# A first MLP layer by Strassen's seven products on three 768-token tiles, with its weights streamed through HBM

## The chip, the cores and the metric

One core of one Trainium2 chip. The metric is the device time of one execution, in microseconds (us). A kernel's time is the median of its runs; one more execution is taken with the hardware profiler.

## The reference

A windowed attention (4 batches, 8 heads of 64, 768 positions, chunks of 32 queries against 8 memory and 56 context keys) gives x of 3072 tokens by 512. Two MLPs follow:

```python
h = np.maximum(np.maximum(x @ w1, x @ w2), x @ w3)     # 512 -> 768
y = h @ w_out                                          # 768 -> 512
h = y @ w_in                                           # 512 -> 2048
g = np.where(h >= 1, h, np.where(h <= -1, 0.0, (h + 1) ** 2 / 4))
out = g @ w_out2                                       # 2048 -> 512
```

All is float32. The kernel splits each operand into a high part of type fp32r and a low part (value minus high part) and takes three matmuls for each product: high-high, low-high, high-low.

## The kernel before

The five engines run their own instruction lists, written out by hand, in order, and meet only in semaphores; nothing is scheduled by a planner.

**Tiles and first MLP.** TT = 384 tokens are a tile, TILES = 8. `tile_a` (TensorE's L541, VectorE's L896, ScalarE's L715) does one tile: for each of six blocks f of 128 hidden columns, three products (w1, w2, w3) of 4 x 3 matmuls each, `layer1` (L495), into the three PSUM banks `mlp[0..2]`. ScalarE copies the first (`h_first`, L699), VectorE takes the maximum with the second and third (L880, L886), ScalarE makes h's high part and VectorE its low part (L892). Then `layer2` (L524): four outputs of 6 x 3 matmuls, copied by ScalarE (`y_out`, L708) and stored to `y_scratch` by SP. All weights of this MLP stay in SBUF. A tile is 216 + 72 matmuls of 384 columns.

**Attention.** 24 groups of 128 tokens. Three are done ahead; each tile of the first seven carries the three groups of the next between its products: `scores` (L449), softmax on VectorE and ScalarE (L839, L858, L674), `transposes` (L460), `weighted_v` (L476), and x's high and low parts straight out of PSUM (L695, L871). q, k and v come in by SP, three groups deep.

**Second MLP.** Tiles of TU = 768 tokens, four of them (u), each with PAIRS = 8 periods: 32 periods g. A period takes one pair of hidden blocks by Strassen: seven products of 2 x 3 matmuls on sums of weight blocks and of y blocks (`product`, L596), alternating between two banks, with the six down-projection outputs of earlier periods between them (`down`, L626: 6 matmuls of 512 columns each). VectorE combines the products (L982 to L1006), ScalarE and VectorE apply the activation and split g (L782, L794, L1008, L1014). y's sums and parts for the next u are made in periods 2 to 6 (L751, L934, L951).

**Weights of the second MLP.** POOL (`split_w_in` L365, `split_w_out` L398) makes the sums and the high and low parts, one item after another through one staging area, while the first MLP runs; SP brings the raw item and stores the result (L271, L278). In the second MLP POOL issues the load of each period's set: `wi` (L416, 1792 KB, two buffers) when the period two before has ended, `wo` (L419, 1024 KB) when its down products have. The loop is L430 to L438.

## Time and profile before

| what | value |
|---|---|
| median of 3 runs | 984.15 us (984.12 to 984.52) |
| profiled execution | 983.69 us |
| its span, first to last instruction | 981.6 us |
| TensorE busy | 968.8 us, 99% |
| VectorE, ScalarE, POOL busy | 48%, 36%, 15% |
| DMA moved | 181.52 MB, 185 GB/s over the span |

The profile books each matmul from its start to a modelled end, and those overlap, so the pace is read from starts. PEld is TensorE's weight load, DVE VectorE, ACT ScalarE, SPq and POOLq the engines as issuers of DMAs. The time outside the span, here 2.1 us, is start and end of the execution.

### The profile page before, as it was taken

What the parts mean: (1) busy time and instruction counts of PE and PEld (TensorE: products, weight loads), DVE (VectorE), ACT (ScalarE), POOL (GpSimd) and SP (SyncE); (2) the same over time, 40 slices, a digit from 0 to 9 for tenths busy, and PEclk for the clock granted to TensorE, in tenths of its full rate; (3) what the DMA queues carried; (4) which work ended last, traced back from release to release, by engine and by line L of the source; (5) the groups of instructions that cost most, each with busy time, mean ns of one, the idle gap of its engine ahead of it and who ended that gap; (6) DMA issues with size and microseconds to landing.
All of it is one profiled execution on the core that took longest, in us unless ns stands there. A gap on an engine that the chain in (4) does not pass through costs nothing.

```text
span 981.6 us, 18566 instructions
## 1 busy us (share of the span) xinstructions
PE 968.8 (99%) x7968; PEld 905.1 (92%) x7968; DVE 469.6 (48%) x713; ACT 354.5 (36%) x553; POOL 150.0 (15%) x176
## 2 busy tenths in 40 slices
PE   6999999999999999999999999999999999999998
PEld 5999999999999999999998888988888888888887
DVE  4662524244252434425456655566545666454452
ACT  3342212222222222222353625545354544444253
POOL 2022442405235230000000000000000000000000
PEclk9999999999999999999999999999999999999999
DMA  9462753645465361042735566655756545575532
GB/s 363 186 234 70 267 183 128 252 144 188 162 236 183 153 231 61 1 172 65 269 131 217 203 220 215 204 196 200 249 191 236 192 161 196 187 258 170 198 118 108
DMA packets 32206, 181.52 MB, mean 185 GB/s; under 512 B 3456, under 2 KB 7552, under 8 KB 21888
## 3 DMA queue, kind: packets, MB, share of 16 engines
q0 software_dynamic: 9216, 92.28, 27.0%
q1 hardware_dynamic: 22912, 88.09, 24.4%
q8 instruction: 63, 1.03, 0.4%
q14 instruction: 15, 0.12, 0.0%
HBM read 144.70 MB, written 35.65 MB: 184 GB/s over the span
## 4 chain that ended last, share of the span: by engine, by line
PE 98%; DMA 1%; DVE 0%; ACT 0%; issue 0%; SPq 0%
PE mlp_ps L491 23%; PE mlp_ps L492 23%; PE mlp_ps L493 23%; PE attn_ps L493 3%; PE scores_ps L493 3%; PE attn_ps L492 3%; PE scores_ps L492 3%; PE attn_ps L491 3%; PE scores_ps L491 3%; PE attn_ps L484 3%; PE scores_ps L457 2%; PE trans_ps L493 2%; PE trans_ps L492 2%; PE trans_ps L491 1%; PE trans_ps L466 1%; DMA qk_raw<-qk_l 1%
## 5 line engine op out<-in xcount | busy, mean ns | idle before, releaser
L491 PE MATMUL mlp_ps<-x_hi,w_hi 128*128 128x384 f32 x572 | 195.1, 341 | 0.0
L493 PE MATMUL mlp_ps<-x_lo,w_hi 128*128 128x384 f32 x572 | 191.5, 335 | 0.0
L492 PE MATMUL mlp_ps<-x_hi,w_lo 128*128 128x384 f32 x572 | 191.2, 334 | 0.0
L492 PE MATMUL mlp_ps<-yc,wi 128*128 128x384 f32 x448 | 150.7, 336 | 0.0
L493 PE MATMUL mlp_ps<-yc,wi 128*128 128x384 f32 x448 | 149.6, 334 | 0.0
L491 PE MATMUL mlp_ps<-yc,wi 128*128 128x384 f32 x448 | 149.6, 334 | 0.0
L787 ACT ACTIVATE ramp<-up,half_col 128x768 f32<-128x768 f32 x64 | 60.1, 939 | 197.4 <-DVE up L1004 178.2
L491 PEld LDWEIGHTS mlp_ps<-x_hi,w_hi 128*128 128x128 f32 x572 | 107.4, 188 | 1.9
L492 PEld LDWEIGHTS mlp_ps<-x_hi,w_lo 128*128 128x128 f32 x572 | 107.5, 188 | 0.0
L493 PEld LDWEIGHTS mlp_ps<-x_lo,w_hi 128*128 128x128 f32 x572 | 107.4, 188 | 0.0
L492 PEld LDWEIGHTS mlp_ps<-yc,wi 128*128 128x128 f32 x448 | 84.1, 188 | 8.8
L491 PEld LDWEIGHTS mlp_ps<-yc,wi 128*128 128x128 f32 x448 | 84.1, 188 | 8.1 <-DVE up L1002 0.3
L672 ACT ACTIVATE h_hi<-h_max 128x384 fp32r<-128x384 f32 x48 | 25.2, 524 | 182.4 <-DVE h_max L889 182.4
L493 PEld LDWEIGHTS mlp_ps<-yc,wi 128*128 128x128 f32 x448 | 84.1, 188 | 0.0
L883 DVE TENSOR_TENSOR h_max<-h_part,mlp_ps 128x384 f32<-128x384 f32 x48 | 26.6, 554 | 106.5 <-PE mlp_ps L493 106.5
L1011 DVE SCALAR_TENSOR_TENSOR ramp<-ramp,up 128x768 f32<-128x768 f32 x64 | 61.1, 955 | 31.9 <-ACT ramp L792 31.9
L417 POOL DMA_DIRECT2D wi<-wi_scratch x32 | 17.1, 533 | 344.0 <-PE mlp_ps L493 295.9
L1016 DVE TENSOR_TENSOR g_hl<-ramp,g_hl 128x768 fp32r<-128x768 f32 x64 | 61.1, 955 | 6.5 <-ACT g_hl L672 5.9
L672 ACT ACTIVATE up<-mlp_ps 128x384 f32<-128x384 f32 x96 | 46.7, 486 | 41.7 <-PE mlp_ps L493 41.7
L491 PE MATMUL mlp_ps<-h_hi,w_out_hi 128*128 128x384 f32 x168 | 56.9, 339 | 0.0
L492 PE MATMUL mlp_ps<-h_hi,w_out_lo 128*128 128x384 f32 x168 | 56.1, 334 | 0.0
L493 PE MATMUL mlp_ps<-h_lo,w_out_hi 128*128 128x384 f32 x168 | 56.1, 334 | 0.0
(138 smaller groups left out, 1653.0 us busy)
## 6 DMA issues: line engine op xcount, KB each, us to landing
wi<-wi_scratch POOLq DMA_DIRECT2D x32, 1792.0 KB, 7.5
wo<-wo_scratch POOLq DMA_DIRECT2D x32, 1024.0 KB, 5.1
qk_raw<-qk_l SPq DMA_DIRECT2D x24, 768.0 KB, 8.1
wi_scratch<-stage_a SPq DMA_DIRECT2D x8, 1792.0 KB, 8.2
v_raw<-v_l SPq DMA_DIRECT2D x24, 512.0 KB, 4.8
wo_scratch<-stage_a SPq DMA_DIRECT2D x8, 1024.0 KB, 6.6
y_scratch<-y_stage SPq DMA_DIRECT2D x32, 192.0 KB, 2.6
y_raw<-y_scratch SPq DMA_DIRECT2D x8, 768.0 KB, 5.3
```

The costliest lines, as they stand in the source:

```text
L417: pool.dma_start(wi[g % 2].rearrange("p h c -> p (h c)"), wi_scratch[g % PAIRS]).then_inc(wi_in[g % 2], 16)
L457: last = pe.matmul(s[part, r, i], q[rows, i, part], k[rows, i, c], start=True, stop=True)
L466: last = pe.transpose(trans_of(n)[:, m * P:(m + 1) * P], prob[:, slot, 2 * m:2 * m + 2], ident[:, :])
L484: last = pe.matmul(o[r * D:(r + 1) * D, i, m, c], v_raw[rows, j, 2 * m + r, c], prob_t_of(n)[rows, 2 * m + r, c], start=True, stop=True)
L491: pe.matmul(out_ap, a_hi, b_hi, start=first, stop=False, skip_group_check=beside)
L492: pe.matmul(out_ap, a_lo, b_hi, start=False, stop=False, skip_group_check=beside)
L493: return pe.matmul(out_ap, a_hi, b_lo, start=False, stop=last, skip_group_check=beside)
L672: return act.activation(o, i, ACT.Copy)
L787: act.activation(ramp[:, f], up[:, g % 2, f].rearrange("p t c -> p (t c)"), ACT.Relu, bias=half_col[:, 0:1], scale=0.5).then_inc(ramp_done, 1)
L883: dve.tensor_tensor(h_max[:, f % 2], h_part[:, :], mlp[1][:, 0:TT], ALU.max).then_inc(h_max2_done, 1)
L1011: dve.scalar_tensor_tensor(ramp[:, f], ramp[:, f], 1.0, up[:, g % 2, f].rearrange("p t c -> p (t c)"), ALU.min, ALU.max).then_inc(g_done, 1)
L1016: dve.tensor_tensor(g_hl[:, g % 2, 1, f], ramp[:, f], g_hl[:, g % 2, 0, f].bitcast(F32), ALU.subtract).then_inc(g_split, 1)
```

## The change

The first two 384-token tiles stay as they were, except that the second carries six attention groups, not three. The other 2304 tokens become three 768-token tiles v. Each has nine periods g (three hidden-block pairs times w1, w2, w3), and a period is seven products of 6 matmuls (Strassen's products in a form where products 2, 4, 5 and 6 add onto a bank that already holds an earlier one, after ScalarE has copied that bank: `snapshot`). VectorE adds and takes the maximum over w1, w2, w3 in SBUF. Every 10th product carries attention for the next tile in the first two of the three. x goes to `x_raw` as float32; `xc_work` on VectorE and `xc_high` on ScalarE make its sums and parts between tiles, and product 0 waits for 6 of the 8 low parts (`x_split`), product 2 for 7, product 6 for all. `l2_product` does the second layer, eight outputs of 18 matmuls per tile.

The first layer's weights for these tiles are 9 items, the second MLP's 8, each of two halves: POOL now loads the raw half, splits it, and stores it (34 halves). Five go through one staging area, the rest through two; 14 are split before the first big tile, then one per period. The sets come back through two `wi` buffers, as in the second MLP, also in the first layer. w_out2 is no longer stored split: POOL loads it raw (512 KB) and splits it in each period. The second MLP uses the same form of the seven products: five ScalarE copies and three VectorE additions per period.

```diff
-TILES = TOKENS // TT
+TILES = 2
...
-W_RAW, W_SUMS, W_COLS = 4 * 2 * P, 5 * 2 * P, 7 * 2 * P
+W_RAW, W_SUMS, W_COLS = 4 * 2 * P, 3 * 2 * P, 7 * 2 * P
+W_HALF = W_COLS // 2
 WO_COLS = 2 * DM
-Y_SUMS, Y_COLS = 5 * TT, 7 * TT
-ITEMS = 2 * PAIRS
-PRODUCTS = (("m1", 0, P, 4), ("m2", 3 * P, 2 * P, 5), ("m5", 2 * P, 2 * P, 6), ("m3", 10 * P, P, 1),
-            ("m4", 12 * P, P, 0), ("m7", 8 * P, P, 3), ("m6", 6 * P, P, 2))
-Y_PARTS = (slice(0, 2 * TT), slice(2 * TT, 4 * TT), slice(4 * TT, 5 * TT), slice(5 * TT, 7 * TT))
-HI_ORDER = (0, 3, 1, 2)
-def build_attention_and_two_mlps(nc, qk_l, v_l, w123, w_out1, w_in2, w_out2, out):
+Y_SUMS, Y_COLS = 3 * TT, 7 * TT
+TILES_S = TILES_B - 1
+KFP = KF1 // 2
+PAIRS_S = 3 * KFP
+PERIODS_S = TILES_S * PAIRS_S
+SLOTS = 7 * PAIRS_S
+GT = 2 * GPT
+ITEMS = PAIRS_S + PAIRS
+EARLY, AHEAD = 5, 14
+Y_ORDER = (0, 3, 1, 2)
+H_ORDER = ((0, 0), (1, 1), (0, 1), (1, 0))
+W_S1, W_A11, W_A12, W_A22, W_S2, W_S3, W_S4 = range(7)
+Y_B11, Y_T3, Y_B21, Y_B22, Y_T1, Y_T2, Y_T4 = range(7)
+PRODUCTS = ((W_A11, Y_B11), (W_A12, Y_B21), (W_S2, Y_T2), (W_S1, Y_T1), (W_S3, Y_T3), (W_S4, Y_B22), (W_A22, Y_T4))
+Y_PARTS = (slice(0, 2 * TT), slice(2 * TT, 4 * TT), slice(4 * TT, 6 * TT), slice(6 * TT, 7 * TT))
+HI_ORDER = (1, 0, 2, 3)
...
+        def staging(n):
+            if n < EARLY:
+                return early_sums[:, :], up_m5[:, 0:W_COLS]
+            start = n % 2 * (W_SUMS // 2 + W_COLS)
+            return (stage_a[:, start:start + W_SUMS // 2], stage_a[:, start + W_SUMS // 2:start + W_SUMS // 2 + W_COLS])
...
+        def l1_bank(g, i):
+            return mlp[(g + (0, 1, 0, 2, 0, 2, 0)[i]) % 3][:, 0:TT]
...
+            for v in range(TILES_S - 1):
+                load_groups(range(GT * (v + 2) + GPT, min(GROUPS, GT * (v + 3) + GPT)))
+                for x in range(2 * KD):
+                    store_part(v, x)
+            sp.wait_ge(x_hi_done, GROUPS)
+            load_y(0, 0)
+            load_y(0, 1)
             load_y(1, 0)
             load_y(1, 1)
-            for d in range(KD):
-                store_y(TILES - 1, d)
+            for x in range(2 * KD):
+                store_part(TILES_S - 1, x)
...
+            def load_raw(n):
+                item, j = divmod(n, 2)
+                src = w_l1[item] if item < PAIRS_S else w_in2[item - PAIRS_S]
+                if n >= 2:
+                    pool.wait_ge(w_split, 2 * (n - 1))
+                pool.dma_start(w_raw[:, n % 2], src[:, j * 4 * P:(j + 1) * 4 * P]).then_inc(raw_in[n % 2], 16)
...
+                pool.tensor_tensor(s3, a11, a21, ALU.subtract).then_inc(w_sums_done, 1)
+                pool.wait_ge(w_sums_done, 4 * n + 1)
+                pool.tensor_tensor(s1, a21, a22, ALU.add).then_inc(w_sums_done, 1)
+                pool.wait_ge(w_sums_done, 4 * n + 2)
+                pool.tensor_tensor(s2, s1, a11, ALU.subtract).then_inc(w_sums_done, 1)
+                pool.wait_ge(w_sums_done, 4 * n + 3)
+                pool.tensor_tensor(s4, a12, s2, ALU.subtract).then_inc(w_sums_done, 1)
+                if n >= EARLY + 2:
+                    pool.wait_ge(w_stored[n % 2], 16 * (n // 2))
+                elif 0 < n < EARLY:
+                    pool.wait_ge(w_stored[(n - 1) % 2], 16 * ((n - 1) // 2 + 1))
+                pool.tensor_copy(hi[:, 0:4 * P], raw).then_inc(w_hi_done, 1)
+                pool.wait_ge(w_sums_done, 4 * n + 4)
+                pool.tensor_copy(hi[:, 4 * P:7 * P], sums).then_inc(w_hi_done, 1)
+                pool.wait_ge(w_hi_done, 2 * n + 1)
+                pool.tensor_tensor(lo[:, 0:4 * P], raw, hi[:, 0:4 * P].bitcast(F32), ALU.subtract).then_inc(w_split, 1)
+                pool.wait_ge(w_hi_done, 2 * n + 2)
+                pool.tensor_tensor(lo[:, 4 * P:7 * P], sums, hi[:, 4 * P:7 * P].bitcast(F32), ALU.subtract).then_inc(w_split, 1)
+                pool.wait_ge(w_split, 2 * (n + 1))
+                if n >= 2:
+                    pool.wait_ge(w_stored[n % 2], 16 * (n // 2))
+                pool.dma_start(wi_scratch[n // 2][:, n % 2 * W_COLS:(n % 2 + 1) * W_COLS], both).then_inc(w_stored[n % 2], 16)
+                if n + 2 < 2 * ITEMS:
+                    load_raw(n + 2)
+            def load_wi(n):
+                item = n % PAIRS_S if n < PERIODS_S else PAIRS_S + (n - PERIODS_S) % PAIRS
+                if n < PAIRS_S or PERIODS_S <= n < PERIODS_S + PAIRS:
+                    for w in w_stored:
+                        pool.wait_ge(w, 16 * (item + 1))
+                pool.dma_start(wi[n % 2].rearrange("p j i x -> p (j i x)"), wi_scratch[item]).then_inc(wi_in[n % 2], 16)
+            load_raw(0)
+            load_raw(1)
+            for n in range(AHEAD):
+                split_half(n)
+            pool.wait_ge(mlp_done, TG + L1G)
+            load_wi(0)
+            load_wi(1)
+            for g in range(PERIODS_S):
+                if AHEAD + g < 2 * ITEMS:
+                    split_half(AHEAD + g)
+                pool.wait_ge(l1_done, 7 * (g + 1))
+                load_wi(g + 2)
...
+            def split_wo(g):
+                pool.wait_ge(wo_raw_in, 16 * (g + 1))
                 if g >= 2:
                     pool.wait_ge(down_done, SUBS * (g - 1))
-                    load_wo(g)
-                pool.wait_ge(prod_done, 7 * (g + 1))
-                load_wi(g + 2)
-            for g in range(PERIODS - 2, PERIODS):
-                pool.wait_ge(down_done, SUBS * (g - 1))
-                load_wo(g)
+                pool.tensor_copy(wo[:, g % 2, 0], wo_raw[:, :, :]).then_inc(wo_hi_done, 1)
+                pool.wait_ge(wo_hi_done, g + 1)
+                for f in range(2):
+                    pool.tensor_tensor(wo[:, g % 2, 1, f], wo_raw[:, f], wo[:, g % 2, 0, f].bitcast(F32),
+                                       ALU.subtract).then_inc(wo_split, 1)
+            pool.wait_ge(l2_done, 2 * KD * TILES_S)
+            load_wo(0)
+            for g in range(PERIODS):
+                split_wo(g)
+                if g + 1 < PERIODS:
+                    pool.wait_ge(wo_split, 2 * (g + 1))
+                    load_wo(g + 1)
+                if g + 2 < PERIODS:
+                    pool.wait_ge(prod_done, 7 * (g + 1))
+                    load_wi(PERIODS_S + g + 2)
...
+            def l1_product(g, i):
+                v, q = divmod(g, PAIRS_S)
+                if i == 0:
+                    pe.wait_ge(wi_in[g % 2], 16 * (g // 2 + 1))
+                if q == 0 and i in (0, 2, 6):
+                    pe.wait_ge(x_split, 8 * v + {0: 6, 2: 7, 6: 8}[i])
+                if i < 2 and q == 0:
+                    pe.wait_ge(y_copied, y_before(v) - 1 + i)
+                elif i < 2:
+                    pe.wait_ge(summed, 3 * g - 2 + 2 * i)
+                elif i == 3:
+                    if q and (q - 1) % 3:
+                        pe.wait_ge(merged, merges(g - 1) + 4)
+                    elif q:
+                        pe.wait_ge(c21_copied, (g - 1) // 3 + 1)
+                else:
+                    pe.wait_ge(snapped, 4 * g + (0, 0, 1, 0, 2, 3, 4)[i])
+                wcols, ycols = (slice(n * c, (n + 1) * c) for n, c in zip(PRODUCTS[i], (P, TT)))
+                w, x = wi[g % 2], yc1
+                begins = i in (0, 1, 3)
+                for j in range(2):
+                    last = three(l1_bank(g, i), (w[:, j, 0, wcols], w[:, j, 1, wcols], x[:, j, 0, ycols], x[:, j, 1, ycols]),
+                                 begins and j == 0, j == 1, not begins)
+                last.then_inc(l1_done, 1)
...
+                for f in range(KF1):
+                    if x == 0 and f in (0, KF1 - 2):
+                        pe.wait_ge(h2_lo_done, 4 * f0 + (3 if f else 0))
+                    if x == 1 and f == KF1 - 1:
+                        pe.wait_ge(h2_lo_done, 4 * f0 + 4)
...
+            def strassen_tile(v):
+                for s in range(SLOTS):
+                    k, r = divmod(s, 10)
+                    n = GT * (v + 2) + k
+                    if v + 1 < TILES_S and r == 0:
+                        if k:
+                            weights_ready(n - 1, (n - 1) % GPT, (n - 1) // GPT)
+                        if k < GT:
+                            scores_ready(n, n % GPT, n // GPT)
+                        if k:
+                            weighted_v(n - 1, (n - 1) % GPT)
+                        if k < GT:
+                            scores(n, n % GPT)
+                    if v + 1 < TILES_S and r == 7:
+                        transposes(n, n % 2)
+                    l1_product(PAIRS_S * v + s // 7, s % 7)
...
+                    pe.wait_ge(summed, 3 * (PERIODS_S - 1) + 1 + 2 * i)
+                elif i == 0:
+                    pe.wait_ge(folded, 3 * g)
+                elif i == 1:
+                    pe.wait_ge(copied, 5 * g)
+                elif i == 2:
+                    pe.wait_ge(copied, 5 * g + 1)
+                elif i == 3:
+                    pe.wait_ge(folded, 3 * g + 1)
                 else:
-                    pe.wait_ge(folded, 6 * g + i - 2)
+                    pe.wait_ge(copied, 5 * g + i - 2)
...
+            def snapshot(g, i):
+                act.wait_ge(l1_done, 7 * g + i + 1)
+                if i == 3:
+                    if g:
+                        act.wait_ge(summed, 3 * g - 1)
+                    copy(m5[:, :], l1_bank(g, i)).then_inc(snapped, 1)
+                    return
+                f, t = {0: (0, 0), 2: (0, 1), 4: (1, 1)}[i]
+                if g and (g - 1) % 3 == 0:
+                    act.wait_ge(summed, 3 * (g - 1) + (1, 0, 3, 0, 2)[i])
+                elif g:
+                    act.wait_ge(merged, merges(g - 1) + (1, 0, 3, 0, 2)[i])
+                if g % PAIRS_S == 0 and i == 0:
+                    act.wait_ge(x_split, 8 * (g // PAIRS_S) + 7)
+                copy(snap[:, f, t], l1_bank(g, i)).then_inc(snapped, 1)
...
+                    if not attention and q in (1, 4):
+                        if i == 5:
+                            yc_high(0, q // 4, HI_ORDER[0:2])
...
+                else:
+                    for w in w_stored:
+                        act.wait_ge(w, 16 * ITEMS)
+                    act.wait_ge(x_split, 8 * TILES_S)
...
+            def xc_work(v):
+                for j in range(2):
+                    for k in range(4):
+                        xc_sum(v, j, k)
+                    for k in HI_ORDER:
+                        xc_low(v, j, k)
```

`down`, `g_values` and `g_high` keep their work. `split_half` begins with the wait for its raw half and names its four blocks of 128 columns a21, a11, a12, a22 and the sums s1 to s4. `yc_sum` makes four differences of 384 columns; in the third big tile it runs at products 2 and 3 of periods 1 and 4, `yc_low` at those of 2 and 5. The eight `y_part` copies follow each `l2_product`.

## Rows read from the trace of the kernel before

**Rows 1.** The page's first part: engine, busy us, share of the span, instructions.

```profile
PE 968.8 (99%) x7968; PEld 905.1 (92%) x7968; DVE 469.6 (48%) x713; ACT 354.5 (36%) x553; POOL 150.0 (15%) x176
```

**Rows 2.** The page's fourth part: the chain that ended last, by engine.

```profile
PE 98%; DMA 1%; DVE 0%; ACT 0%; issue 0%; SPq 0%
```

**Rows 3.** TensorE's timeline in tile 2: start us, duration us, engine, line, operation.

```profile
143.07 0.33 PE L491 MATMUL mlp_ps<-x_hi,w_hi 128*128 128x384 f32 x1
...
148.27 0.33 PE L491 MATMUL mlp_ps<-x_hi,w_hi 128*128 128x384 f32 x1
```

**Rows 4.** Table by stretch, tile 1: length, busy per engine (count), PEclk, DMA share, GB/s.

```profile
84.06:141.72 57.66, 57.66 (x692) 56.16 (x698) 21.70 (x40) 13.11 (x25) 19.67 (x19) 1.00 0.53 193
```

**Rows 5.** Timelines of TensorE and POOL where a period of the second MLP ends.

```profile
606.06 0.33 PE L493 MATMUL mlp_ps<-yc,wi 128*128 128x384 f32 x1
...
606.69 0.53 POOL L417 DMA_DIRECT2D wi<-wi_scratch  x1 [7.81 <-PE mlp_ps L493]
...
622.33 0.53 POOL L417 DMA_DIRECT2D wi<-wi_scratch  x1 [7.82 <-PE mlp_ps L493]
```

**Rows 6.** Timeline: a product's last matmul, and ScalarE's copy of it.

```profile
611.96 0.33 PE L493 MATMUL mlp_ps<-yc,wi 128*128 128x384 f32 x1
...
612.34 0.49 ACT L672 ACTIVATE up<-mlp_ps 128x384 f32<-128x384 f32 x1 [1.21 <-PE mlp_ps L493]
```

**Rows 7.** Timeline of the start: a ScalarE copy and the weight load waiting for it.

```profile
12.62 0.60 ACT L672 ACTIVATE prob_t<-trans_ps 128x512 f32<-128x512 f32 x1 [2.34 <-PE trans_ps L466]
...
13.28 1.82 PEld L484 LDWEIGHTS attn_ps<-prob_t,v_raw 64*64 64x64 f32 x64 [1.10 <-issue]
```

**Rows 8.** Groups by line and shape: count, busy us, mean ns, idle before, releaser.

```profile
L672 ACT ACTIVATE up<-mlp_ps 128x384 f32<-128x384 f32 x96 | 46.7, 486 | 41.7 <-PE mlp_ps L493 41.7
...
L410 POOL TENSOR_TENSOR stage_a<-stage_b,stage_a 128x512 fp32r<-128x512 f32 x16 | 20.3, 1291 | 0.6
...
L1004 DVE TENSOR_TENSOR up<-up,mlp_ps 128x384 f32<-128x384 f32 x32 | 17.7, 554 | 39.1 <-PE mlp_ps L493 39.0
...
L960 DVE TENSOR_TENSOR yc<-y_sums,yc 128x768 fp32r<-128x768 f32 x16 | 15.1, 951 | 0.0
...
L672 ACT ACTIVATE yc<-y_sums 128x768 fp32r<-128x768 f32 x16 | 13.4, 840 | 6.9 <-DVE y_sums L942 4.7 <-DVE y_sums L946 2.2
...
L406 POOL CAST stage_a<-stage_b 128x1024 fp32r<-128x1024 f32 x8 | 8.8, 1104 | 120.9 <-DMA wi_scratch<-stage_a 120.9
...
L375 POOL TENSOR_TENSOR stage_a<-stage_b 128x256 f32<-128x256 f32 x8 | 5.8, 731 | 43.0 <-DVE w_out_lo L878 41.9
```

**Rows 9.** DMA issues: count, KB each, median us from issue to landing; last, wi's range.

```profile
wi<-wi_scratch POOLq DMA_DIRECT2D x32, 1792.0 KB, 7.5
wo<-wo_scratch POOLq DMA_DIRECT2D x32, 1024.0 KB, 5.1
qk_raw<-qk_l SPq DMA_DIRECT2D x24, 768.0 KB, 8.1
...
v_raw<-v_l SPq DMA_DIRECT2D x24, 512.0 KB, 4.8
...
DMA to landing us min/median/max: 7.2/7.5/10.6
```

**Rows 10.** Table by stretch, columns as in rows 4: the loads at the start.

```profile
3.00:17.00 14.00, 8.31 (x267) 6.79 (x268) 9.80 (x20) 4.88 (x7) 1.81 (x1) 1.00 1.02 415
```

**Rows 11.** TensorE's timeline at the start: first matmuls of 384 columns.

```profile
22.85 0.52 PE L510 MATMUL mlp_ps<-x_hi,w_hi 128*128 128x384 f32 x1
...
24.13 0.52 PE L510 MATMUL mlp_ps<-x_hi,w_hi 128*128 128x384 f32 x1
```

**Rows 12.** Timelines of VectorE and POOL: one subtract alone, one beside a POOL cast.

```profile
90.65 0.56 DVE L894 TENSOR_TENSOR h_lo<-h_max,h_hi 128x384 fp32r<-128x384 f32 x1 [0.59 <-ACT h_hi L672]
...
120.10 1.25 POOL L387 CAST stage_a<-stage_a 128x1280 fp32r<-128x1280 f32 x1
...
120.61 1.15 DVE L894 TENSOR_TENSOR h_lo<-h_max,h_hi 128x384 fp32r<-128x384 f32 x1 [0.59 <-ACT h_hi L672]
```

814 lines of the change are left out of this document (514 added, 300 removed).

## The prediction

> **What bounds the kernel now.** I read four views in this order. The page's first part and its chain: TensorE is busy for 99% of the span and carries 98% of the chain that ended last [rows 1, 2]. So time falls only where TensorE gets fewer instructions, and any new wait of TensorE is paid in full. Second, TensorE's timeline: from 143.07 to 148.27 stand 30 matmuls of 384 columns, one each 0.1733 us, though each is booked at 0.33 us [rows 3]: they are pipelined, and the pace is the price. Third, the stage table: a tile takes 57.66 us, 288 x 0.1733 = 49.9 of it matmuls, so 7.75 for three attention groups, 2.58 each [rows 4]. DMA is then only half busy at 193 GB/s. Fourth, the second MLP's period is 15.64 us, between two loads of a weight set [rows 5]: 42 products' matmuls of 0.1733, and 36 down matmuls that share the rest, 0.232 each. That is the cover every stream has there.
>
> **Part 1: fewer matmuls.** Six 384-token tiles cost 216 first-layer matmuls each; three 768-token tiles cost 9 pairs x 7 products x 6 = 378. 1296 - 1134 = 162 go, x 0.1733 = **-28.1 us**. Second layer (576), attention (24 groups), second MLP (1344 and 1152) keep their counts. A first-layer period (42 products) is then 7.28 us; in the first two of the three tiles six groups are spread over nine periods, 6/9 x 2.58 = 1.72 more: 9.00 us.
>
> **Part 2: hand-overs inside a period.** Products 2, 4, 5 and 6 each need a ScalarE copy made one product earlier; nothing else lies between. ScalarE starts 0.38 after the last matmul's start (611.96 to 612.34), copies 0.486, and TensorE's weight load follows a ScalarE end by 0.06 (12.62 + 0.60 to 13.28) [rows 6, 7]: 0.93. It is due six matmuls later, 1.04. The margin is 0.11, so an idle ScalarE hides it. Exponents, transposes' copies and high parts stand in other slots, and where one overlaps it costs tenths; VectorE's softmax likewise. With no row that shows it, the bounds are 0 and 8; I take **+2.0**, near the low end, since the computed margins are positive. At the last product of the first two big tiles, the low parts (VectorE max, ScalarE copy, VectorE subtract, twice in line) are 0.6 later than the four-pass cover of the first output: 2 x 0.6 = **+1.2**.
>
> **Part 3: start of the first big tile.** TensorE has the 72 second-layer matmuls, 12.5 us, plus weighted_v. Behind the last group stand eight sums and six low parts on VectorE before x_split reaches 6: 8 x 0.55 + 5 x 0.95 + 0.55 and the ScalarE hand-overs, about 11 [rows 8]. The two load sets are issued when the 14th half is split. Five halves wait singly for the store before (about 9.3 each from 31 us: casts and subtracts 3.4, issue 0.5, landing 5.1), nine take about 7, ending near 141; the set lands by 149, when TensorE comes. Bounds 0 and 8 (below, rival C); I take **+1.0**. That products begin after part of x rather than all saves here the 1.5 of the last two low parts.
>
> **Part 4: the stream, the largest unknown.** Two weight buffers: set g+2 is issued when period g ends and must be in when g+1 ends. POOL wakes 0.63 after the last matmul's start (606.06 to 606.69), landing takes 7.5 (7.2 to 10.6) [rows 5, 9], and 0.06 back: 8.19. A late set gives the next one that much more room, so a period stretches to (8.19 + own length)/2: half of the excess is lost.
> In the **third big tile** 7.28 is 0.91 short: every second period waits, about three times outside the store's wait below: **+2.7**.
> In the **first two** 9.00 seems enough, but the set shares the DMA engines. Per period: 1.835 MB of set, 0.917 MB store and 0.262 MB raw of one half, and 6/9 of a group's 1.311 MB: 3.89 MB, 432 GB/s. At the start 14 us ran at 415 with the share at 1.02 [rows 10]. So 9.37 at least: 0.37 x 14 periods (seven per tile have a set in their way) = 5. The set also queues in POOL's ring behind the store. Low bound 0 (landing 7.2, traffic smoothed over the second layers), high bound 23.8 (rival S); I take 0.5 a period, **+7.0**, nearest to the byte floor.
> POOL itself: four adds of 128 columns (0.45 by the line through 256 and 512), subtracts 1.01 and 1.29, casts 0.6 and 0.5, dependent waits 0.6: 5.8; two issues 0.53 each, one for the set: 7.5 a period against 9.00 [rows 5, 8]. Its cover is thin, 1.5; gone, the set's issue is late one for one. SP loses the 32 raw and split transfers; it keeps attention, y and out. Its y loads stand ahead of the last tile's stores, which nobody waits for soon.
>
> **Part 5: a new wait in the third big tile.** ScalarE's first yc copy (period 1, after product 5) waits until all 34 halves are stored. Half 33 is split only in that period: issue at 1.16 after its start, split 5.8, then a store. It is bounded by the landing of 512 and 1024 KB, 4.8 and 5.1 [rows 9]: it lands at 12.2. Behind the waiting ScalarE are two wide copies (0.84 each) and period 2's first snapshot; TensorE's product 2 of period 2 comes at 14.5 instead of 9.36: **+5.1**, less if the store is quicker, bounds 3 and 7. What comes after the stall: at the start of the kernel, after sparse work, matmuls ran at 0.32 apart instead of 0.173, the lower of TensorE's two levels, for 4 us [rows 11]; if the wait drops it, 12 matmuls lose 1.8. Half a chance: **+0.9**.
> The Trainium skill ("TensorE: Matmul & The Clock Gate", Part 1) says that a long enough idle puts the array back to 1.2 GHz; the trace here has no idle of this length after its start.
>
> **Part 6: second MLP.** Down matmuls (6 x 0.232 = 1.39) stand between products, so the same copy has 1.5 us of margin. ScalarE gets two copies more (1.0), VectorE three narrow adds instead of two wide and four narrow ones. POOL now splits w_out2: cast 1.10 and two subtracts 1.29, 3.7 per period, behind down_done in mid-period, due 12 us later; each wo load is halved. All hidden by the 15.64; were it gone, 32 periods would pay. **0**. In tile 0 five stores and raw loads join the weights' loading at half DMA load: 0.
>
> **The sum.** -28.1 + 2.0 + 1.2 + 1.0 + 2.7 + 7.0 + 5.1 + 0.9 = -8.2. The profiled execution took 983.69 (span 981.6 and 2.1 around it), so 975.5; the runs' median, 984.15, is 0.46 above it: 976.0.
>
> **Rivals.**
> F, the stream hides: landings stay near 7.5, store wait 4. -28.1 + 1 + 4 + 2.7 + 1.2 + 0.5 = -18.7: 965.4. For it: 0.5 DMA share now. Against: 3.89 MB in 9.00 us.
> S, the other side: the set stands in POOL's ring behind its store and raw load (2.8 us at 415 GB/s) and shares with a group (3.2, half of it): landing 7.5 + 2.8 + 1.6, about 11.7 with the response 12.4. 14 x (12.4 - 9.0)/2 = 23.8 in place of 7.0: 992.8. It decides from an average landing of 10.5, where the term is 15.7 and eats the rest; 10.6 is the largest of 32 [rows 9].
> The Trainium skill ("DMA: Bandwidth & Descriptors", Specifications) limits one core's HBM traffic to 358 GB/s; by that a period would be 10.9, 14 x 1.9 = 26, and the time about 995. Rows 10 speak against it.
> C, VectorE and POOL collide: a subtract with both inputs in SBUF takes 0.56 and, beside a POOL cast, 1.15 [rows 12]. All 14 conversions ahead of the first big tile are such, and POOL splits beside them: 14 x 0.6 = 8.3 instead of 1.0: 983.3. Against: POOL pauses between operations.
> The Trainium skill ("SBUF — State Buffer", Who interferes with whom) says such an instruction and a POOL one that reads SBUF exclude each other for its whole length.
> H, the 0.11 margin is not there: 27 x 4 hand-overs x 0.11 = 11.9 instead of 2: 986. Against: both rows behind 0.93.
> N, the change does not do what it says: x's last parts or the wi set are late, so that the early start gains nothing: 1.5 more, 977.5.
>
> **How the numbers follow.** Forecast 0.47, F 0.20, S 0.18, C 0.07, H 0.05, N 0.03. The range leaves out about a tenth on each side: 965 to 993; the forecast's own is 970 to 982. A measurement of this kernel tells 0.2% (2 us) from no change. Faster: forecast, F, N and some of C: 0.72; same 0.06; slower: S, H: 0.22.
>
> **What would show it.** TensorE's idle, now none after 22 us, should appear (a) before weight loads at starts of periods, released by the set's DMA, alternate ones in the last big tile at 0.9; (b) once, about 5 us, behind a ScalarE snapshot in the third tile's period 2, with ScalarE waiting for the store; (c) about 0.6 ahead of the fifth step of the first output. The set's median landing should be 8 to 9.5 in big tiles. A 384-column pace other than 0.1733, idle before products 2, 4, 5, 6 throughout, or landings over 10.5 prove me wrong.

## The result, and the profile after

The changed kernel takes 1016.67 us (median of 4 runs, 1013.46 to 1021.69) against 984.13 for the kernel before on the same chip: a ratio of 1.0336 (95% interval 1.0289 to 1.0384), so slower by 3.4%. The forecast was 976.0, in a range of 965 to 993: wrong in sign and outside the range. The profiled execution took 1021.69 us, with a span of 1019.9 against 981.6. It is the slowest of the four, 5 us above the median, so what is counted in its trace explains 38.3 us between spans, where the medians lie 32.5 apart.

The page of the changed kernel, busy time and parts of the timeline (40 slices of 25.5 us):

```profile
PE 958.8 (94%) x7806; PEld 888.4 (87%) x7806; DVE 479.6 (47%) x728; ACT 440.5 (43%) x722; POOL 419.4 (41%) x535
...
PE   5999975988998989899999999999999999999998
...
POOL 2768994766628473300033232332332323323321
PEclk9999996997999889999999999999999999999999
```

Against [rows 1] TensorE has 162 matmuls fewer, as the change says, yet the span grew. In slices 6 to 17 it is no longer full, and its clock dips in several of the same slices. POOL went from 15% to 41% of the span, and is at nine tenths in slices 5 and 6. TensorE's waits (total us, times, longest):

```profile
PE mlp_ps L561 <- DMA wi<-wi_scratch: 38.8, 10, 18.1
PE mlp_ps L561 <- ACT up_m L827: 5.6, 4, 4.0
...
PE mlp_ps L561 <- DVE up_m L1432: 0.9, 1, 0.9
```

Before there was no wait at all behind the start. The table by stretch, whose columns are those of [rows 4]: the wait at the start of the first big tile, that tile's first periods, the rest of it, the second layer, the second big tile, its second layer, the third:

```profile
149.00:165.00 16.00, 0.11 (x1) 0.11 (x1) 1.56 (x4) 0.00 (x0) 11.84 (x19) 0.55 0.86 298
165.00:186.00 21.00, 21.00 (x223) 20.58 (x224) 8.38 (x17) 6.61 (x13) 7.71 (x13) 0.86 0.70 255
186.00:262.00 76.00, 67.56 (x882) 63.97 (x881) 46.65 (x76) 26.21 (x53) 52.70 (x76) 0.91 0.95 355
262.00:296.00 34.00, 33.88 (x253) 33.22 (x253) 21.68 (x33) 13.47 (x24) 9.41 (x11) 1.00 0.57 201
296.00:386.00 90.00, 80.72 (x1068) 76.19 (x1068) 50.43 (x87) 30.39 (x61) 59.86 (x88) 0.91 0.82 305
386.00:418.00 32.00, 31.88 (x184) 31.56 (x183) 17.58 (x24) 12.88 (x23) 8.86 (x10) 1.00 0.50 178
418.00:480.00 62.00, 54.22 (x297) 52.62 (x296) 36.26 (x64) 23.79 (x47) 10.67 (x16) 0.97 0.71 252
```

The reader sees two losses here. One is TensorE's idle: 16, 8, 9 and 8 us. The other is PEclk, the granted clock, below 1 behind each long wait. After 165 us the time lost to the clock in the four stretches under 1.00 is 21 x 0.14 + 76 x 0.09 + 90 x 0.09 + 62 x 0.03 = 19.7 us, of which some fell on idle time; following the clock's records, TensorE worked at the lower level for 36.3 us in all, 18 us lost. In the second layers (262 to 296, 386 to 418) the DMA engines are about half idle: a supply that is not used.

The timeline of POOL and TensorE around the largest wait:

```profile
153.49 0.57 POOL L459 DMA_DIRECT2D wi_scratch<-stage_a  x1 [0.99 <-POOL stage_a L455]
154.06 0.54 POOL L424 DMA_DIRECT2D w_raw<-w_l  x1
154.59 1.08 POOL L468 DMA_DIRECT2D wi<-wi_scratch  x2
...
164.89 0.69 PE L561 MATMUL mlp_ps<-yc,wi 128*128 128x384 f32 x1 [18.10 <-DMA wi<-wi_scratch]
165.37 0.52 PE L562 MATMUL mlp_ps<-yc,wi 128*128 128x384 f32 x1
165.69 0.52 PE L563 MATMUL mlp_ps<-yc,wi 128*128 128x384 f32 x1
```

The two first sets are issued at 154.59, because POOL first finishes its 14 splits; they hold the first four halves alone, the last of which was stored at 74.16, and their buffers were free from about 135 us (where the first experiment issues them). The matmuls behind the wait are 0.32 apart. How long a set took to land (from the start of its issue to its last byte), issued in the first big tile from 186 us, in the second and in the third, is in the view of wi's loads by stretch:

```profile
DMA to landing us min/median/max: 7.5/10.7/11.9
...
DMA to landing us min/median/max: 7.5/10.4/12.3
...
DMA to landing us min/median/max: 7.4/7.8/9.3
```

It was 7.2/7.5/10.6 before [rows 9]. The third tile's long wait, ScalarE and TensorE:

```profile
431.03 1.57 ACT L827 ACTIVATE yc<-y_raw 128x768 fp32r<-128x768 f32 x2 [6.70 <-DMA wi_scratch<-stage_a]
...
433.04 0.45 PE L561 MATMUL mlp_ps<-yc,wi 128*128 128x384 f32 x1 [3.96 <-ACT up_m L827]
```

The second MLP is as it was, 15.64 us from one load to the next, as in [rows 5]:

```profile
551.17 0.53 POOL L468 DMA_DIRECT2D wi<-wi_scratch  x1 [3.97 <-PE mlp_ps L563]
...
566.81 0.53 POOL L468 DMA_DIRECT2D wi<-wi_scratch  x1 [3.96 <-PE mlp_ps L563]
```

The balance: 981.6 - 28.1 (matmuls) + 45.9 (TensorE's idle behind 30 us, gaps of more than 0.15) + 18 (clock) = 1017.4. Two smaller terms belong to it. The idle is booked from a matmul's modelled end, 0.33 behind its start, where the next could have started after 0.173, so each of the 17 gaps costs about 0.16 more: 2.7 in all, an estimate. And this execution left its start earlier: TensorE's 201st matmul of 384 columns began at 64.01, in the kernel before at 65.28 (the clock rose at 17.3 and at 26.5): -1.3. That makes 1018.8, and 1.1 of 1019.9 is left. So the expected gain was there; the waits and their echo in the clock are more than twice as large. The question for the experiments is what makes the waits: the place of the loads in POOL's queue (theory P), the room, that is, the time between a buffer coming free and the moment its new contents are needed (M), or the bytes (B).

### The profile page after: what moved, and what is told of

It is laid out like the page before. It is cut to its first block and busy times, and to the rows that moved or that the text cites. A ratio compares the mean times of both kernels' runs of the same rounds, so it can differ in the third digit from the quotient of the medians.

```text
span 1019.9 us, 18893 instructions
## 1 busy us (share of the span) xinstructions
PE 958.8 (94%) x7806; PEld 888.4 (87%) x7806; DVE 479.6 (47%) x728; ACT 440.5 (43%) x722; POOL 419.4 (41%) x535
## 3 DMA queue, kind: packets, MB, share of 16 engines
q1 hardware_dynamic: 18304, 56.63, 15.7%
## 5 line engine op out<-in xcount | busy, mean ns | idle before, releaser
L561 PE MATMUL mlp_ps<-yc,wi 128*128 128x384 f32 x826 | 286.4, 347 | 45.6 <-DMA wi<-wi_scratch 38.8
L827 ACT ACTIVATE up_m<-mlp_ps 128x384 f32<-128x384 f32 x302 | 147.6, 490 | 345.1 <-PE mlp_ps L563 338.9
L562 PE MATMUL mlp_ps<-yc,wi 128*128 128x384 f32 x826 | 282.7, 342 | 0.0
L563 PE MATMUL mlp_ps<-yc,wi 128*128 128x384 f32 x826 | 281.5, 341 | 0.0
L561 PEld LDWEIGHTS mlp_ps<-yc,wi 128*128 128x128 f32 x826 | 159.2, 193 | 60.6 <-DMA wi<-wi_scratch 42.2
L562 PEld LDWEIGHTS mlp_ps<-yc,wi 128*128 128x128 f32 x826 | 159.5, 193 | 8.8
L563 PEld LDWEIGHTS mlp_ps<-yc,wi 128*128 128x128 f32 x826 | 159.2, 193 | 0.0
L1438 DVE SCALAR_TENSOR_TENSOR ramp<-ramp,up_m 128x768 f32<-128x768 f32 x64 | 61.5, 961 | 112.4 <-ACT ramp L1095 112.4
L1090 ACT ACTIVATE ramp<-up_m,half_col 128x768 f32<-128x768 f32 x64 | 60.0, 937 | 69.4 <-DVE up_m L1432 66.8
L494 POOL TENSOR_TENSOR wo<-wo_raw,wo 128x512 fp32r<-128x512 f32 x64 | 84.3, 1333 | 2.7
L827 ACT ACTIVATE g_hl<-ramp 128x768 fp32r<-128x768 f32 x64 | 53.8, 840 | 10.1 <-DVE ramp L1438 10.1
L1095 ACT ACTIVATE ramp<-ramp 128x768 f32<-128x768 f32 x64 | 53.8, 840 | 1.0
L563 PE MATMUL attn_ps<-wo,g_hl 128*128 128x512 f32 x128 | 50.8, 397 | 0.0
L563 PE MATMUL scores_ps<-wo,g_hl 128*128 128x512 f32 x128 | 50.8, 397 | 0.0
L562 PE MATMUL attn_ps<-wo,g_hl 128*128 128x512 f32 x128 | 50.5, 395 | 0.0
L562 PE MATMUL scores_ps<-wo,g_hl 128*128 128x512 f32 x128 | 50.5, 395 | 0.0
```

Source lines behind the costliest of these rows:

```text
L494: pool.tensor_tensor(wo[:, g % 2, 1, f], wo_raw[:, f], wo[:, g % 2, 0, f].bitcast(F32), ALU.subtract).then_inc(wo_split, 1)
L561: pe.matmul(out_ap, a_hi, b_hi, start=first, stop=False, skip_group_check=beside)
L562: pe.matmul(out_ap, a_lo, b_hi, start=False, stop=False, skip_group_check=beside)
L563: return pe.matmul(out_ap, a_hi, b_lo, start=False, stop=last, skip_group_check=beside)
L827: return act.activation(o, i, ACT.Copy)
L1090: act.activation(ramp[:, f], up[:, g % 2, f].rearrange("p t c -> p (t c)"), ACT.Relu, bias=half_col[:, 0:1], scale=0.5).then_inc(ramp_done, 1)
```

## The experiments

Ten more kernels were run, each against the kernel before on the same chip. Medians, ratios to the kernel before with 95% intervals, and TensorE's idle behind 30 us in the profiled run:

| kernel | us | ratio | idle |
|---|---|---|---|
| changed kernel | 1016.67 | 1.0336 (1.0289 to 1.0384) | 45.9 |
| e1, first sets by SP | 1006.60 | 1.0226 (1.0198 to 1.0255) | 33.9 |
| e2, matmuls in the first wait | 1017.57 | 1.0326 (1.0281 to 1.0371) | 28.3 |
| e3, e1 without the second MLP's splits | 991.77 | 1.0092 (1.0068 to 1.0116) | 26.7 |
| e7, e1 with POOL's loads ahead of its splits | 1004.39 | 1.0197 (1.0178 to 1.0216) | 34.5 |
| e8, all sets by SP, whole | 994.54 | 1.0096 (1.0077 to 1.0116) | 23.2 |
| e4, all sets by SP, in two parts | 978.67 | 0.9952 (0.9935 to 0.9968) | 16.3 |
| e10, e8 with the splits spread | 987.94 | 1.0037 (1.0017 to 1.0058) | 23.3 |
| e5, e4 with the splits spread | 965.30 | 0.9814 (0.9797 to 0.9831) | 6.8 |
| e6, e5 with three splits in the third tile | 971.21 | 0.9858 (0.9835 to 0.9881) | 9.5 |
| e11, e5 with four y stores by ScalarE | 965.57 | 0.9832 (0.9796 to 0.9868) | 4.2 |

**The first sets by SP (e1).** Its semaphores for these two loads are new ones.

```diff
             load_groups(range(GT + GPT, 2 * GT + GPT))        # SP
+            sp.wait_ge(mlp_done, TG + L1G)
+            load_set(0)
+            load_set(1)
             for d in range(KD):
                 store_y(1, d)
...
-            pool.wait_ge(mlp_done, TG + L1G)                  # POOL
-            load_wi(0)
-            load_wi(1)
```

> The first two sets of the first big tile are issued by SP (once layer 1 of the second 384-token tile is done, 137 us in the changed kernel) instead of by POOL behind its 14 splits (154.59 us). Theory P (the place in POOL's queue made the 18.10 us wait): TensorE waits at most 4 us there, for the conversions of x, which end near 150.5 us; its clock does not fall for long; time 1016.7 - 18 to 21, so 995 to 999. Rival T (the transfers were the limit: at 137 us they share the rings with the last half stores): the sets land at 155 us or later, the wait is 8 us or more, and the time is 1006 or more. The later waits for wi and the 3.96 us of the third tile should stay as they are under both.

1006.6 us: 10 us gained, not 18 to 21 (theory P had said 995 to 999). Before the first product TensorE waits 0.60 us in place of 18.10. But the third set shows what the first had hidden (timelines of POOL and TensorE):

```profile
166.59 0.54 POOL L477 DMA_DIRECT2D wi<-wi_scratch  x1
...
166.77 0.34 PE L569 MATMUL mlp_ps<-yc,wi 128*128 128x384 f32 x1
176.60 0.69 PE L567 MATMUL mlp_ps<-yc,wi 128*128 128x384 f32 x1 [9.49 <-DMA wi<-wi_scratch]
```

The two sets landed at 145.4 and 151.5, so rival T is out for them. POOL, still at its splits up to 166 (the fourteenth half, with the sets in flight, was stored at 158.56 instead of 153.49), issued the third set 10 us after its buffer came free (period 0 ended near 156.5), and that set took 10 us to land. Half of the first wait had only been moved. Theory P is right on the place and was too short in reach.

**Matmuls in the wait (e2).**

```diff
             second_tile()
+            pe.wait_ge(prob_t_done, 2 * GT)
+            for _ in range(NFILL):                            # 33
+                for _ in range(3):
+                    pe.matmul(trans_ps[:, 0:TT], w_out1_hi[:, 0:P], h_hi[:, 0], start=True, stop=True)
             for v in range(TILES_S):
```

> 99 matmuls of 384 columns into an idle bank are issued by TensorE in the wait at the start of the first big tile (99 x 0.173 = 17.2 us of its 18.1); the sets still land at the same time. It adds work and removes none. Theory K (the clock falls because TensorE stands idle): the low stretch from 150.4 to 170.9 us goes, the matmuls after the wait are 0.173 apart from the first on, and the time falls by about 3 us against the changed kernel (1013.5) although TensorE does more. Rival (the clock falls for the load of the other engines or by its own schedule): matmuls after 165 us are still 0.32 apart for some us and the time is unchanged or higher.

TensorE's timeline where the fill ends:

```profile
163.30 0.69 PE L749 MATMUL trans_ps<-h_hi,w_out_hi 128*128 128x384 f32 x3
...
166.44 0.44 PE L562 MATMUL mlp_ps<-yc,wi 128*128 128x384 f32 x1 [1.67 <-DMA wi<-wi_scratch]
166.72 0.34 PE L563 MATMUL mlp_ps<-yc,wi 128*128 128x384 f32 x1
166.90 0.34 PE L564 MATMUL mlp_ps<-yc,wi 128*128 128x384 f32 x1
167.07 0.34 PE L562 MATMUL mlp_ps<-yc,wi 128*128 128x384 f32 x1
```

The matmuls are 0.17 apart from the start, not 0.32. From the first product of the tile to the next mark, the hand-over wait in the third period, TensorE took 189.97 - 166.44 = 23.5 us, in the changed kernel 191.18 - 164.89 = 26.3. So the idle is what lowered the clock, and the low level cost 2.8 us here. The span of the profiled execution fell by 2.1 us (1019.9 to 1017.8), although everything in it is 1 us late from the start on (the first half is stored at 40.29, in the changed kernel at 39.34). The median did not move (1017.57): the changed kernel's runs lie 8 us apart (1013.5 to 1021.7) and e2's 10 (1011.2 to 1021.0), too far for a gain of 3 us to be seen in them. The Trainium skill ("TensorE: Matmul & The Clock Gate", Part 1) says that a long enough idle puts the array back to its lower clock, and this pair of traces agrees.

**Without the second MLP's splits (e3).** POOL's splits and stores end with the fourth big period. The second MLP then runs on the first MLP's sets, so this kernel's output is not the reference's; its traffic there is the same.

```diff
-                if AHEAD + g < 2 * ITEMS:
+                if AHEAD + g < 2 * PAIRS_S:
                     split_half(AHEAD + g)
...
-                item = n % PAIRS_S if n < PERIODS_S else PAIRS_S + (n - PERIODS_S) % PAIRS
+                item = n % PAIRS_S if n < PERIODS_S else (n - PERIODS_S) % PAIRS
```

> On top of the run with SP's sets: the 16 halves of the second MLP's weights are neither split nor stored (its periods load the first MLP's eight first sets in their place, so its output is of other weights). POOL then does nothing from the fourth big period on but issue set loads, and the store traffic ends there. Theory Q (the halves made the stream late): from the fifth big period on no wait for wi in the first two big tiles is above 0.5 us, the 3.96 us wait in the third tile is gone, the third tile's waits under 1 us may stay (set landing 7.5 against its 7.3 us period); the idle sum falls by 16 to 18 us beyond the first wait and the clock gives 10 or more: 965 to 972. Rival (a set's own landing is the limit, halves or not): waits of some us stay in the first two big tiles, and the time is above 985.

991.77 us, in the rival's range (above 985) and far from theory Q's 965 to 972, though Q was right on the store wait. 14.8 us came from e1's 1006.6: the store wait in the third tile is gone, the waits of 3.06, 4.26, 3.81 and 2.02 us are now 2.50, 2.15, 1.93 and none. What is left, with the landings from 186 to 262 us:

```profile
PE mlp_ps L567 <- DMA wi<-wi_scratch: 21.2, 8, 10.1
...
DMA to landing us min/median/max: 7.3/7.8/9.9
```

10.1 is the third set again, behind the split. The rest are single loads: of the seven issued from 186 to 262 us two landed in 9.55 and 9.89 us, where the limit is 9.00 - 0.63 = 8.4, and the two waits there stand behind them. The last half's store (199.37) was issued in the last 2.2 us of the slower one, the other had no half in its way. Loads of an attention group were in flight beside both (from 189.4 and 218.1); whether they are the cause was not tried. So neither theory alone: the halves cost about 15 us, and without them the stream still has no room.

**POOL's loads first (e7).** On top of e1:

```diff
-                if AHEAD + g < 2 * ITEMS:
-                    split_half(AHEAD + g)
                 pool.wait_ge(l1_done, 7 * (g + 1))
                 load_wi(g + 2)
+                if AHEAD + g < 2 * ITEMS:
+                    split_half(AHEAD + g)
```

> On top of the run with SP's first sets: POOL issues the load of a period's end before it splits that period's half, not behind it, so no load is later than the split that runs at that moment. In the run without this the third set was issued at 166.59 us for a period that ended near 158, and TensorE waited 9.49. Theory P (the loads are late in POOL's queue): issue near 159, wait at most 2 us there, the other waits of 3 to 4 us down to 1 to 2: time 990 to 996. Rival B (the transfer queue is what is slow): landings of 10 us stay, waits of 2 us at many period starts in place of a few long ones, time 998 to 1004.

1004.39 us, 2 under e1, which is within the scatter of both, and at the rival's upper end (998 to 1004). The third set's wait fell from 9.49 to 2.94, and waits for wi from 26.0 to 19.0 in all. But every half is now later by a period, and the third tile's wait for the last store grew (ScalarE, TensorE):

```profile
414.97 1.58 ACT L835 ACTIVATE yc<-y_raw 128x768 fp32r<-128x768 f32 x2 [13.49 <-DMA wi_scratch<-stage_a]
...
416.97 0.69 PE L567 MATMUL mlp_ps<-yc,wi 128*128 128x384 f32 x1 [10.94 <-ACT up_m L835]
```

4.16 became 10.94, and ate 7 us. On this one queue loads and splits pushed each other; landings stayed at 7.6/10.8/12.0.

**Sets in two parts, by SP (e4), and whole, by SP (e8).** The edit of e4 (e8 has one load per set, after product 6). Not shown: in both, SP takes attention's and y's loads in the same list, each at a fixed product, where the changed kernel issues them as soon as their buffers are free.

```diff
+            def load_part(n, h):                              # SP
...
+                if n >= 2:
+                    sp.wait_ge(l1_done, 7 * (n - 2) + (4, 7)[h])
+                cols = slice(0, 3 * P) if h == 0 else slice(3 * P, 7 * P)
+                src = wi_scratch[item].rearrange("p (j i x) -> p j i x", j=2, i=2)[:, :, :, cols]
+                sp.dma_start(wi[n % 2][:, :, :, cols].bitcast(F32), src).then_inc(wi_part_in[n % 2][h], 16)
...
-                if i == 0:                                    # TensorE
-                    pe.wait_ge(wi_in[g % 2], 16 * (g // 2 + 1))
+                if i in (0, 2):
+                    pe.wait_ge(wi_part_in[g % 2][i // 2], 16 * (g // 2 + 1))
```

> All splits and stores as in the changed kernel, but each set is loaded by SP in two parts: the three blocks of products 0, 1, 3 once product 3 of the period two before is done, the other four after product 6, needed only at product 2; so no load waits for POOL, and each has 11.5 us or more to land in place of 8.4. Theory M (only the margin of a load and its place in POOL's queue are missing; the bytes fit): waits for wi nearly all under 0.5 us, sum of idle under 8 us, of it about 4 us the wait for the y store if that stays: 962 to 975. Rival B (the bytes are the limit: 3.89 MB per 9.00 us period takes 9.37 at 415 GB/s): about 0.4 us per period with a half is left, 6 to 7 us of waits in the two big tiles plus the clock: 980 to 988.

> As the run with two-part loads by SP (978.67 us), but each set is loaded by SP whole, after product 6 of the period two before, so it has the 9.0 us of one period to land. It tells the place in POOL's queue (removed here too) from the margin of a load (kept as in the changed kernel). Theory P alone (POOL's queue was it): within 3 us of 978.67. Theory M (the margin matters as much): landings of 9 to 11 against 8.4 to 9.0 leave waits of 1 to 2 us at most starts of a period in the first two big tiles and about 0.5 in the third, 20 us and more in all: 995 to 1003.

978.67 and 994.54 us. e4 is 0.5% under the kernel before with all of the change's traffic in it; it came out between theory M's range (962 to 975) and B's (980 to 988). Taking the loads out of POOL's queue, together with SP's new order, is worth 12 us (1006.6 to 994.5); the two were not separated. Giving each load more room, by two parts, is worth another 16. That is theory M, as e8 expected, at the low end of its 995 to 1003, but with seven waits of up to 4.49 us, 14.3 in all, and not small ones at most periods. In e4's table by stretch the bytes come to light:

```profile
149.00:194.00 45.00, 39.22 (x574) 36.57 (x572) 29.96 (x49) 15.75 (x32) 38.23 (x56) 0.99 1.03 401
194.00:235.00 41.00, 40.79 (x513) 39.62 (x514) 26.91 (x46) 16.10 (x33) 27.84 (x41) 0.93 1.01 381
...
235.00:262.00 27.00, 26.87 (x155) 26.55 (x155) 17.43 (x24) 11.27 (x20) 10.16 (x13) 1.00 0.73 279
```

For 45 us the DMA engines are full at 401 GB/s, parts land in 9.3/12.1/15.5 us, and the room of 11.5 is used up at 194, where TensorE waits 3.77. In the second layer behind it they are not full.

**The splits spread (e5, and e10 with whole sets).** Six halves in the first big tile, three in each second-layer stretch, eight in the second tile.

```diff
+SPLIT_PERIODS, SPLIT_WINDOW = (0, 2, 4, 5, 7, 8, 9, 10, 11, 12, 13, 14, 15, 17), 3
...
             for g in range(PERIODS_S):
-                if AHEAD + g < 2 * ITEMS:
-                    split_half(AHEAD + g)
+                if g in SPLIT_PERIODS:
+                    split_half(n)
+                    n += 1
                 pool.wait_ge(l1_done, 7 * (g + 1))
+                if g % PAIRS_S == PAIRS_S - 1 and n < 2 * ITEMS:
+                    pool.wait_ge(l2_done, 2 * KD * (g // PAIRS_S) + 2)
+                    for _ in range(SPLIT_WINDOW):
+                        split_half(n)
+                        n += 1
```

> As the run with two-part loads by SP, but the 20 halves left are spread: six in the first big tile instead of nine, three in each second-layer stretch between the tiles, where the transfers idle, and eight in the second tile; none in the third. Theory B' (with the margin there, what is left of the waits is bytes: nine halves in a row at 402 GB/s): the 3.77 us wait in the first tile goes and with it 3.4 us of its low clock; the 3.93 us wait behind the store of y in the third tile goes, since all halves are stored before it; the second tile's 3.30 may stay, with its eight halves: 965 to 970. Rival: waits of the same size elsewhere, 975 or more.

> The fourth corner of a table of two by two: sets loaded whole by SP (994.54 us with the changed kernel's split schedule) together with the spread schedule of the halves (965.3 us with sets in two parts). If the two edits add up (each gives back its own share of the waits): 994.5 - 13.4 = 981, waits of about 1 us at many period starts. If few bytes are enough (theory B'): 970 or less, since landings come down to 7 to 8 us. If the margin is what counts (theory M): 988 or more.

e5 takes 965.3 us, 1.9% under the kernel before. Its waits, and its table over the same times as the changed kernel's. The stages lie earlier here (second big tile 257 to 339 us, third 365 to 430), so the rows show how full TensorE and the DMA engines are, and not the same stage:

```profile
PE trans_ps L567 <- DVE prob L1219: 4.0, 2, 2.6
PE mlp_ps L594 <- ACT up_m L863: 1.4, 3, 0.8
```

```profile
186.00:262.00 76.00, 76.00 (x906) 73.86 (x905) 48.59 (x82) 31.17 (x60) 49.57 (x72) 1.00 0.90 333
262.00:296.00 34.00, 33.32 (x455) 31.51 (x454) 23.03 (x37) 13.39 (x28) 29.09 (x44) 1.00 1.02 387
296.00:386.00 90.00, 89.31 (x909) 87.56 (x902) 58.20 (x95) 37.77 (x72) 46.91 (x64) 1.00 0.85 302
```

In these stretches TensorE is all but full and the clock at its upper level, and in the whole run only one wait for wi above 0.15 us is left (0.69 at 298). The wait behind the last store, 3.93 in e4, is gone. e10 takes 987.9 us. The table of two by two:

| | splits as in the change | splits spread | spread gives |
|---|---|---|---|
| sets whole | 994.5 | 987.9 | 6.6 |
| in two parts | 978.7 | 965.3 | 13.4 |
| parts give | 15.9 | 22.6 | |

The two do not add up; each gives more with the other. With whole sets the median landing came down to 8.0 (9.6 in e8), and ten waits for wi, 18.9 us, are still there (e10's landings from 186 to 262 us, and its waits for wi): the worst landing of each few counts, not the median. That is nearest to theory M's number (988). TensorE's idle is the same in both profiles (23.2 and 23.3); most of what e10 gained over e8 stands in the clock, 12.2 us of work at the lower level in place of 22.7.

```profile
DMA to landing us min/median/max: 7.3/8.0/11.6
```

```profile
PE mlp_ps L590 <- DMA wi<-wi_scratch: 18.9, 10, 4.0
```

**Three halves in the third tile (e6).** The expectation says four of the second tile's halves; the kernel moves three (periods 18 to 20), and issues the second pair of y loads three periods later. What waits for the last half, the first y's conversion, moves three periods later.

```diff
-                        if q in (1, 4):
+                        if q in (4, 7):
                             for part in (2 * i - 4, 2 * i - 3):
-                                yc_sum(0, q // 4, part)
+                                yc_sum(0, q // 7, part)
```

> As the spread run, but four of the second big tile's halves go to the third tile, which has no attention, and what must wait for the last half (the conversion of the second MLP's first y) moves three periods later. Theory B': no wait for wi above 0.5 us in any tile, no 3.9 us behind a store: 959 to 964, near 984 - 28.1 + 1.2 + 1.5 = 959. Rival: in the third tile a period of 7.3 us with a set and a half moves 3.0 MB (411 GB/s), so waits of 1 to 3 us come up there: 965 to 970.

971.21 us, just above the rival's range (965 to 970) and 6 more than e5. TensorE waits 3.08 us at 387.2. The table by stretch of e6 there:

```profile
375.00:395.00 20.00, 16.57 (x78) 15.93 (x77) 8.31 (x13) 4.35 (x9) 15.68 (x23) 0.83 1.02 388
```

The last of the second layer's three halves, those of the first periods, two y loads and the sets of a 7.3 us period meet; parts took up to 12.99 us, and the wait of 3.08 stands behind that one. So the third tile had no room for these halves, though it has no attention.

**The y stores by ScalarE (e11).**

```diff
-            for d in range(KD):                               # SP
-                store_y(1, d)
...
+            def store_y1(d):                                  # ScalarE, behind each y_out(1, d)
+                act.wait_ge(y_copied, 2 * KD + d + 1)
+                act.dma_start(y_scratch[:, d, TT:2 * TT], y_stage[:, d]).then_inc(y_stored[d], 16)
```

> As the spread run, but the four stores of y of the second 384-token tile are issued by ScalarE on its own queue instead of by SP behind the first sets. In the spread run VectorE waits 4.8 us for such a store (block sums of the first period), the softmax of group 12 is late behind it, and TensorE waits 2.63 us at 156.24 and runs 3.4 us at the low clock. Theory V (those stores stand behind the sets in SP's ring): the 2.63 us wait goes, 965.3 - 2.6 - 1.5 = 961 to 962.5. Rival (VectorE is late for its work beside POOL's splits): the wait stays above 2 us and the time at 965.

In e5's timeline of VectorE stands what it was to remove:

```profile
153.87 0.55 DVE L1342 TENSOR_TENSOR up_m<-up_m,mlp_ps 128x384 f32<-128x384 f32 x1 [4.78 <-DMA y_scratch<-up_m]
```

It did in the profile: TensorE's softmax wait of 2.63 us is gone, a wait of 0.79 stands in its place, and the clock does not fall. The span is 961.4 (e5: 962.8), and this execution's start, ahead of anything that the edit touches, was 2.3 us slower (TensorE's 201st matmul of 384 columns at 65.52 against 63.17), so behind it e11 gained 3.7 us, near the forecast 4.1. So theory V holds for TensorE's wait, but only in part for the stores: the last of them, now on ScalarE's queue, still took 9.28 us, landing beside the last part of the second set (157.53 and 157.49), and VectorE waits 2.80 us for it. The median, 965.57, does not show it: its four runs lie from 963.2 to 971.1, and the interval of the ratio takes in e5's. Whether e11 is faster than e5 stays open.

## Why the prediction was wrong

**Part 1 (-28.1): right.** 7968 - 7806 = 162 matmuls, and e5 is 18.6 us below the kernel before (983.92 beside it) with 6.8 us of idle and 3.4 us of work at the lower clock left.

**Part 2 (+2.0, +1.2): right in size.** ScalarE hand-overs above 0.15 us show twice in the big tiles (0.42 and 0.40), behind two other copies in a row; with the 1.1 us that the balance leaves over, they come to about 2. The +1.2 at the first output did not show: no gap above 0.15 us stands there. Rival H is out.

**Part 3 (+1.0): the first step that failed.** The sentence was that nine halves take "about 7, ending near 141". The stores of the halves in the changed kernel's view of that tile (first and last start):

```profile
L459 POOL DMA_DIRECT2D wi_scratch<-stage_a x9: 562/562/571, 89.7 to 153.5; - x9
L459 POOL DMA_DIRECT2D wi_scratch<-up_m x5: 562/562/562, 39.3 to 82.6; - x5
```

The first five ended at 82.6, where 31 + 5 x 9.3 gives 77.5; the nine took 70.9 / 9 = 7.9 each. Seven of them took 7.3 each (82.6 to 133.9), the last two 10.3 and 9.3, beside VectorE's conversions of x (134.0 to 149.0). The same cast and the same subtract just ahead of these conversions, and beside them:

```profile
130.35 0.61 POOL L449 CAST stage_a<-w_raw 128x512 fp32r<-128x512 f32 x1
131.37 1.28 POOL L453 TENSOR_TENSOR stage_a<-w_raw,stage_a 128x512 fp32r<-128x512 f32 x1
138.92 1.34 POOL L449 CAST stage_a<-w_raw 128x512 fp32r<-128x512 f32 x1
141.00 1.59 POOL L453 TENSOR_TENSOR stage_a<-w_raw,stage_a 128x512 fp32r<-128x512 f32 x1
```

So of the 12 us by which the fourteenth half was late, about 5 are this collision, and 5 were there with the fifth half already. The worse error is that I priced the landing and not the place: the sets stand behind all 14 splits in POOL's queue, though they need four halves. A slip of 12 us there is paid one for one. It cost 18.1 us of waiting and 2.8 of clock (e2); e1 shows that the cure of this place alone brings 10, since the third set, issued behind the fifteenth split, waits next.

**Part 4: the mechanism was right, the size was not.** In the third tile the waits for wi are 0.81, 0.90, 0.68 and 1.43, 3.8 us for a forecast of 2.7. In the first two tiles I took 7.0. There were five waits, 4.55, 3.47, 3.85, 0.78 and 4.25 us, 16.9 in all. The forecast named a median landing of 8 to 9.5; it was 10.7 and 10.4. Rival S had said that it decides from an average of 10.5, "where the term is 15.7": the term came out at that size with medians about there, though the averages were only 10.0 and 9.8, since a few loads landed in 7.5. The four long waits stand behind landings of 10.9 to 12.3. S was given 0.18. I held the byte floor (9.37 us a period at 415 GB/s) for the nearest row, but a floor with all engines full is not what a period gets: the changed kernel moved 355 and 305 GB/s in these tiles and still waited, since a set has to be in by a fixed moment. That it is slowed by the store and the group under way is likely and was not separated. e8 and e4 differ only in how a set is loaded, whole or in two parts with more room, and that is worth 16 us. POOL's lateness, "its cover is thin, 1.5; gone, the set's issue is late one for one", was written down and put at nothing. Another order in POOL's queue gave 2 us (e7, not clear of the scatter), SP's queue with its new order of loads 12 (e8).

**The clock: the term that was missing.** I priced its fall once, for half a chance, at 0.9. It fell behind six waits, and 36.3 us of work ran at the lower level: 18 us, where the largest cost in my sum was 7.0. Every wait had to be priced with its echo: behind the five of 3.5 to 4.6 us TensorE worked for 3.4 to 9.5 us at about half its pace, so a wait of 4 us costs 5.7 to 8.8. Rival S, at 992.8, lacked the same term.

**Part 5 (+5.1 and +0.9): right.** 3.96 us of waiting and 1.7 of clock, where half a chance of 1.8 was in the sum. The store landed in 4.6 us. It goes when the halves are stored earlier (e5), and grows when they come later (e7).

**Part 6 (0): right.** 15.64 us a period before and after. At its first period three waits of 0.79, 0.88 and 0.45 came up, 2.1 us in all, that I did not have.

**Rival C** had the wrong victim. VectorE's conversions were late by little: in e1 TensorE waits 0.60 us for them, not 8.3. But the two engines do slow each other, and POOL's splits paid for it, with the 5 us of part 3. The limit of 358 GB/s, the other rival on that side, is out as well: e4 moved 401 GB/s for 45 us. The Trainium skill ("HBM Reference", Specifications (TRN2)) says that a core that streams alone gets more than that share, and the trace agrees.

**The sum again, with measured terms:** -28.1 + 18.1 (first sets) + 16.9 and 3.8 (stream) + 4.8 (ScalarE waits in big tiles) + 2.3 (around the second MLP's start) + 18 (clock) + 2.7 (booking of the gaps) - 1.3 (earlier start) + 1.1 (left over) = +38.3, the difference of the spans.

What stays open: why the landings of a set have a median near 10.5 us at a mean of only 305 to 355 GB/s. The order of transfers within one queue and the sharing among queues were not separated.

## What to carry to other kernels

Where a kernel is bound by one full engine, price each stream by the worst landing that it may meet and by its place in the issuing queue, not by the mean of the bytes: ask what the issuing engine is doing at the moment when the buffer comes free. Buy room before bandwidth: split a load along the order in which its parts come free and are needed, issue it from a queue that has nothing long in it, and put background work where the transfers idle. And add to each wait of TensorE of 2 us or more a price for the clock behind it: in these eleven profiles the waits of 2.0 to 4.6 us lost, by half of the work at the lower level, about 0.7 of their own length again.
